# Who makes the low parts of the channel weights: VectorE or GpSimd, in a fused attention, gMLP and mixer kernel

## The chip, the cores and the metric

One NeuronCore of a Trainium2 chip. The metric is the device time of one launch in microseconds (us). Both versions take the same inputs and compute the same outputs.

## The reference, cut to what matters

Three stages follow each other over 4 batches of 576 tokens. The change touches the last half of the last one, and the end of the one before it.

```python
# 1: windowed attention, 8 heads of 64 -> x [4, 576, 512]
# 2: gMLP (moe_*), gives x again as [4, 576, 512]
# 3: mixer (moe2_*)
xt = x.transpose(0, 2, 1)
h = np.maximum(xt @ w_tok1, 0.0) @ w_tok2           # token layers: 576 -> 256 -> 576
u = x + h.transpose(0, 2, 1)
h2 = np.maximum(u @ w_ch1, 0.0) @ w_ch2             # channel layers: 512 -> 1536 -> 512
return (u + h2).astype(np.float32)                  # the residual is u
```

## The kernel before, in words

**Products in three passes.** A float32 operand is kept as two float32r parts: the high part is a rounded copy that ScalarE makes, the low part is the raw value minus the high one. A product is three matmuls (high by high, high by low, low by high), `product` in the code.

**Stages.** Attention, gMLP and the token layers run batch by batch, by orders written out by hand for each engine (`PROLOGUE_`, `FIRST_`, `LOOP_`, `EPILOGUE_`). In them `b00` to `b31` are the eight pieces of the second token layer, and `te` is VectorE's addition of x to a piece. VectorE then transposes the sum in 32 by 32 blocks (`ut0` to `ut3`), and SyncE stores it twice: `st` as it is, for the channel layers' input, and `sr` as rows, for the final residual (four issues for each of four pieces).

**The channel stage.** It runs over the 2304 tokens in NS = 3 spans of 768, and in each span over NI = 6 blocks of hidden channels, so NW = 18 rounds n = 0 to 17; s and i are the span and the block of round n. A round has seven first products P0 to P6 (`first_product`, six matmuls of 128x384 each). They are a Strassen-like scheme: seven products of sums of quarters in place of eight. Then there are twelve second products (`second_product`, three matmuls of 128x512 each), which add into six PSUM banks over the six rounds of a span. TensorE runs the first products of round n and puts the second products of round n - 1 behind them, 2, 2, 2, 1, 2, 2 and 1 of them after P0 to P6 (`AFTER_SLOT`).

**What each round needs.** SyncE loads the channel weights: `load_weights(n + 1)` (three issues, first product, waits for P6 of round n - 1) and `load_second(n)` (one issue, second product). VectorE's `weight_sums` makes four sums of quarters (L1162 to L1167), ScalarE's `weight_high` (L879) the high parts of all seven, 1792 elements per partition, and `second_high` (L883) those of the second weights, 1024 elements. GpSimd makes the low parts: `second_low` (L729, 1024) and `weight_low` (L725, 1792). For the next span's tokens, `data_sum` (VectorE), `data_high` (ScalarE) and `data_low` (GpSimd, L718, 768 elements) do the same, seven times per span.

**The products' results.** PSUM bank 6 is copied out by ScalarE (`copy_part` 0, 1, 2, L887, after P0, P2, P4), and VectorE's `add_part` 0, 1, 2 (L1173) adds bank 7 to such a copy. P3 waits for `add_part` 0, P6 for `add_part` 1, P1 of the next round for `add_part` 2. P2, P4 and P5 each wait for a `copy_part`. ReLU and the split into high and low parts are `hidden_high` j (ScalarE, L895, L899) and `hidden_low` j (VectorE, L1178), j = 0 to 3. P0 of the next round waits for `hidden_low` 2, since it writes the same bank.

**The end of a span.** At i = 0 the six output tiles of the span before are ready one after the other. `add_rest` r to r + 5 (VectorE, L1187) adds the residual rows to a tile, SyncE's `store` writes it out and `load_rest` fetches the next residual rows into one of three buffers; those of r + 3, r + 4 and r + 5 are loaded only after `add_rest` of r, r + 1 and r + 2. The second products of the new span start each bank anew, so the first of them waits for `add_rest` r + 3, the second for r + 4, the third for r + 5.

**The order.** Each engine runs its instructions in program order, so an instruction that waits holds all behind it on its engine. SyncE issues all DMAs, in one order too.

## Time and profile before

| | us |
|---|---|
| median of 3 runs | 674.92 |
| lowest, highest | 674.79, 676.52 |
| the profiled execution | 676.68 |
| its span, first to last instruction | 674.7 |

| engine | busy, share of the span |
|---|---|
| TensorE | 643.8 us, 95% |
| VectorE | 403.8 us, 60% |
| ScalarE | 297.8 us, 44% |
| GpSimd | 272.9 us, 40% |

### The profile page before, as it was taken

What the parts mean: (1) busy time and instruction counts of PE and PEld (TensorE: products, weight loads), DVE (VectorE), ACT (ScalarE), POOL (GpSimd) and SP (SyncE); (2) the same over time, 40 slices, a digit from 0 to 9 for tenths busy, and PEclk for the clock granted to TensorE, in tenths of its full rate; (3) what the DMA queues carried; (4) which work ended last, traced back from release to release, by engine and by line L of the source; (5) the groups of instructions that cost most, each with busy time, mean ns of one, the idle gap of its engine ahead of it and who ended that gap; (6) DMA issues with size and microseconds to landing.
All of it is one profiled execution on the core that took longest, in us unless ns stands there. A gap on an engine that the chain in (4) does not pass through costs nothing.

```text
span 674.7 us, 11567 instructions
## 1 busy us (share of the span) xinstructions
PE 643.8 (95%) x3917; PEld 590.7 (88%) x3917; DVE 403.8 (60%) x1026; ACT 297.8 (44%) x733; POOL 272.9 (40%) x279
## 2 busy tenths in 40 slices
PE   5999999999999999999999789999899999899995
PEld 5898999999999999999999678998788989789893
DVE  4987977578766786656645366445665435344422
ACT  4965357334563354633363235543244543333320
POOL 3551536412153121541058034686153776154310
PEclk9999999999999999999999889999999999999998
DMA  9868144585436863347211731324522323522314
GB/s 203 204 113 184 32 131 125 125 175 122 120 95 133 182 129 91 102 130 153 86 32 39 218 103 63 110 63 164 194 63 62 111 63 93 173 63 62 110 32 140
DMA packets 190873, 77.49 MB, mean 115 GB/s; under 512 B 127328, under 2 KB 177056, under 8 KB 190816
## 3 DMA queue, kind: packets, MB, share of 16 engines
q1 hardware_dynamic: 190816, 76.76, 44.1%
q8 instruction: 32, 0.52, 0.3%
q14 instruction: 25, 0.20, 0.1%
HBM read 55.49 MB, written 21.23 MB: 114 GB/s over the span
## 4 chain that ended last, share of the span: by engine, by line
PE 84%; DMA 4%; DVE 4%; issue 3%; SPq 2%; ACT 1%; POOL 0%; DVEq 0%; POOLq 0%
PE ps L1277 59%; PE ps L1378 13%; PE ps L1347 5%; PE ps L1317 5%; DMA front<-in_moe_w_ch_dram 1%; DMA early<-u_rows 1%; PE ps L1441 1%; SPq L579 1%; DMA xT<-u_scratch 1%; DVE arena L1178 1%; DVE att L1001 1%; PE ps L1327 1%; DVE front L1187 0%; ACT xT L887 0%; DVE att L1154 0%
## 5 line engine op out<-in xcount | busy, mean ns | idle before, releaser
L1277 PE MATMUL ps<-arena 128*128 128x288 f32 (+3 forms) x2100 | 399.2, 344 | 4.2 <-ACT xT L887 2.6
L1277 PEld LDWEIGHTS ps<-arena 128*128 128x128 f32 (+1 forms) x2100 | 336.0, 187 | 40.1 <-issue 5.2
L1277 PE MATMUL ps<-att_r,arena 128*128 128x384 f32 x504 | 102.3, 339 | 9.7 <-ACT xT L887 5.8
L1277 PEld LDWEIGHTS ps<-att_r,arena 128*128 128x128 f32 x504 | 90.5, 189 | 18.7 <-issue 11.9
L729 POOL TENSOR_TENSOR arena<-front,arena 128x1024 fp32r<-128x1024 f32 x18 | 44.3, 2458 | 146.7 <-ACT arena L883 146.7
L687 POOL TENSOR_SCALAR att<-att,rinv 128x128 f32<-128x128 f32 x144 | 53.2, 389 | 97.9 <-DVE rinv L1012 97.7
L1378 PE MATMUL ps<-arena 128*128 128x288 f32 (+1 forms) x560 | 89.6, 316 | 0.0
L1378 PEld LDWEIGHTS ps<-arena 128*128 128x128 f32 x560 | 80.5, 188 | 4.1
L725 POOL TENSOR_TENSOR arena<-front,arena 128x1792 fp32r<-128x1792 f32 x18 | 74.7, 4149 | 0.0
L1173 DVE TENSOR_TENSOR vr<-ps,xT 128x384 f32<-128x384 f32 x36 | 20.0, 556 | 87.2 <-ACT xT L887 54.0
L789 ACT ACTIVATE att<-att,nmax 128x128 f32<-128x128 f32 x144 | 56.0, 391 | 25.0 <-DVE nmax L1001 24.4
L899 ACT ACTIVATE arena<-vr 128x384 fp32r<-128x384 f32 x36 | 18.9, 526 | 67.2 <-PE ps L1277 46.1
L1178 DVE SCALAR_TENSOR_TENSOR arena<-vr,arena 128x384 fp32r<-128x384 f32 x36 | 40.3, 1121 | 9.7 <-ACT arena L899 9.7
L887 ACT ACTIVATE xT<-ps 128x384 f32<-128x384 f32 x54 | 26.2, 485 | 42.0 <-PE ps L1277 41.9
L1001 DVE CUSTOM_DVE_ANT_0 att<-ps,mask 128x128 f32<-128x128 f32 x144 | 33.1, 285 | 10.7 <-PE ps L1317 10.1
L718 POOL TENSOR_TENSOR att_r<-att,att_r 128x768 fp32r<-128x768 f32 x14 | 26.8, 1933 | 30.9 <-DVE att L1157 30.9
L1317 PE MATMUL ps<-att 128*128 128x128 f32 x288 | 37.5, 280 | 1.2 <-DVE att L975 1.2
L1347 PE MATMUL ps<-att 128*128 128x128 f32 x288 | 36.9, 276 | 0.7 <-DVE att L975 0.4
L1317 PEld LDWEIGHTS ps<-att 128*128 128x128 f32 x288 | 35.5, 197 | 1.6 <-DVE att L975 1.4
L693 POOL TENSOR_TENSOR rstd<-veps,mhalf 128x1 f32<-128x1 f32 (+1 forms) x20 | 12.7, 637 | 58.3 <-DVE veps L1077 58.3
L1347 PEld LDWEIGHTS ps<-att 128*128 128x128 f32 x288 | 34.8, 192 | 1.4 <-DVE att L975 0.6
L799 ACT ACTIVATE xT<-ps 64x256 f32<-64x256 f32 x72 | 27.1, 376 | 14.6 <-PE ps L1347 13.6
(98 smaller groups left out, 665.9 us busy)
## 6 DMA issues: line engine op xcount, KB each, us to landing
front<-in_moe_w_ch_dram SPq DMA_DIRECT2D x18, 512.0 KB, 4.8
prob_blocks<-att SPq DMA_DIRECT2D x27, 256.0 KB, 2.5
att<-prob_blocks SPq DMA_DIRECT2D x108, 64.0 KB, 2.0
u_scratch<-uy SPq DMA_DIRECT2D x16, 288.0 KB, 2.8
front<-in_moe_w_ch_dram SPq DMA_DIRECT2D x18, 256.0 KB, 2.9
front<-in_moe_w_ch_dram SPq DMA_DIRECT2D x36, 128.0 KB, 3.3
early<-u_rows SPq DMA_DIRECT2D x18, 256.0 KB, 4.5
att<-in_v_dram SPq DMA_DIRECT2D x16, 256.0 KB, 3.8
```

Source lines behind the costliest of these rows:

```text
L687: ins = pool.tensor_scalar(x, x, rinv[:, g % 3, p:p + 1], 1.0, ALU.mult, ALU.mult)
L718: pool.tensor_tensor(x_at[s % 2][:, c, 1], x_raw[s % 2][:, c, 1], x_at[s % 2][:, c, 0].bitcast(F32), ALU.subtract) \
L725: pool.tensor_tensor(a_lo_at[n % 2], a_raw[n % 2], a_hi_at[n % 2].bitcast(F32), ALU.subtract).then_inc(a_lo, 1)
L729: pool.tensor_tensor(w2_lo_at[n % 2], w2_raw[n % 2], w2_hi_at[n % 2].bitcast(F32), ALU.subtract).then_inc(w2_lo, 1)
L789: ins = act.activation(x, x, ACT.Exp, bias=nmax[:, g % 3, p:p + 1], scale=-1.0, accum_out=psums[:, g % 3, p:p + 1])
L799: ins = act.activation(xT3[c, :, blk * WINDOW:(blk + 1) * WINDOW], tp[c, bank, :].rearrange("p (w h n) -> p w h n", w=PAIRS, h=2)[:, :, h, ...
L1001: ins = dve.tensor_tensor_reduce(out=prob[:, g % 3, P * p:P * (p + 1)], in0=ps[:, 4 + g % 2, P * p:P * (p + 1)], in1=mask[:, 0:P] if blk e ...
L1178: dve.scalar_tensor_tensor(out=h_at[:, j, 1], in0=src, scalar=0.0, in1=h_at[:, j, 0].bitcast(F32), op0=ALU.max, op1=ALU.subtract).then_inc ...
L1277: ins = pe.matmul(dst, w[a], x[c], start=first and n == 0, stop=last and n == 2, skip_group_check=True)
L1317: ins = pe.matmul(ps[:, 4 + g % 2, P * p:P * (p + 1)], qd[:, g // 2 % 2, g % 2, p].rearrange("p h n -> p (h n)"), kT[:, p, at:at + P], sta ...
L1347: ins = pe.matmul(tp[:, bank, P * p:P * (p + 1)], window[:, P * p:P * (p + 1)], keys[:, p], start=True, stop=True)
L1378: ins = pe.matmul(dst, d, w, start=t == 0 and n == 0, stop=t == NT - 1 and n == len(pairs) - 1, skip_group_check=True)
```

## The change

1. `weight_low` and `second_low` of rounds from 1 on (for the weights of rounds from 2 on) go from GpSimd to VectorE, with semaphores of their own (`a_low`, `w2_low`). GpSimd keeps `data_low`, and in the opening the low parts of the first weights.
2. Within a round the order on VectorE and ScalarE is written anew: `second_high` stands behind `copy_part` 2 rather than ahead of `copy_part` 1; `hidden_low` 0 stands ahead of `weight_sums`; `data_sum` comes one block later (i = 2, 3) and `data_high` is spread as 2, 2, 2 and 1; `add_rest` comes later in the round at i = 0.
3. At the end of the last batch (`EPILOGUE_`), TensorE puts P2 to P6 of round 0 between the pieces b of the second token layer rather than behind them, and VectorE and ScalarE follow; the transposes `ut` come last on VectorE.
4. SyncE issues the second weights of round 1 (`cw41`) ahead of the stores `st3`, and the first weights of round 2 (`ca42`) behind them but ahead of the row stores `sr3`. Before, both came after all stores, in the loop.

The diff:

```diff
--- before.py
+++ after.py
@@ -67,7 +67,7 @@
         "V7 V8 b21 v2 + b31 v3 + v4 + u00 + u10 + u20 + u30 + u01 + u11 + u21 + u31 +").split()
     EPILOGUE_PE = (
         "g00 + g10 + g20 + g30 + g01 + g11 + g21 + g31 + y00 + y10 + y20 + y30 + y01 + t0 t1 y11 + y21 + y31 + a0 "
-        "t2 t3 a1 t4 a2 a3 a4 P0 P1 b00 b10 b20 b30 b01 b11 b21 b31 P2 P3 P4 P5 P6").split()
+        "t2 t3 a1 t4 a2 a3 a4 P0 P1 b00 P2 b10 P3 b20 P4 b30 b01 P5 b11 P6 b21 b31").split()
     PROLOGUE_ACT = (
         "qe0 qe1 e0 e1 qe2 e2 e3 o0 e4 o1 xh0 qe3 o2 e5 e6 wh0 o3 xh1 ze4 wh1 wh2 o4 e7 o5 e8 xh2 vr0 vr1 wh3 o6 "
         "o7 xh3 uu00 vh0 vr2 uu10 o8 uu20 xh4 vh1 vh2 uu30 wh4 vr3 vr4 wh5 vh3 uu01 vh4 uu11 uu21 uu31").split()
@@ -81,7 +81,7 @@
         "uu20 uu30 uu01 uu11 vh4 uu21 uu31").split()
     EPILOGUE_ACT = (
         "gh00 gh10 gh20 gh30 ae0 gh01 xe0 gh11 yy00 xe1 yy10 yy20 gh21 gh31 xe2 yy30 xe3 yy01 th0 th1 xe4 yy11 "
-        "yy21 xe5 yy31 we0 th2 th3 th4 ae1 xe6 ah0 ah1 pc0 pc1 pc2 he0 he1 he2 he3").split()
+        "yy21 xe5 yy31 we0 th2 th3 th4 ae1 xe6 ah0 ah1 pc0 he0 pc1 pc2 he1 he2 he3").split()
     PROLOGUE_DVE = (
         "ke0 m0 vo1 m1 r0 ke1 ke2 r1 m2 c0 hu0 m3 r2 c1 m4 vo2 r3 c2 m5 ke3 hv0 hv1 hv2 r4 c3 m6 xl0 lv0 hu1 hv3 "
         "c4 r5 r6 lv2 m7 wl0 c5 m8 xl1 vo3 r7 wl1 wl2 c6 xl2 hu2 r8 hu3 c7 vs0 vs1 wl3 vo4 vn0 xl3 c8 vl0 vn1 vs2 "
@@ -99,8 +99,8 @@
         "te30 te01 vn0 vs1 te11 vl0 te21 te31 vn1 ut0 vs2 ut1 vl1 vn2 vs3 vl2 vn3 ut2 ut3 vs4 kt0 vl3 vn4 kt1 vl4").split()
     EPILOGUE_DVE = (
         "sa00 sm00 gl00 sa10 sm10 gl10 sa20 sm20 sa30 gl20 as0 sm30 xs0 gl30 sa01 sa11 sm01 gl01 sm11 sa21 gl11 "
-        "sa31 xs1 sm21 sm31 xs2 gl21 gl31 as1 xs3 tl0 tl1 tl2 tl3 tl4 al0 al1 cs0 te00 te10 te20 te30 te01 te11 "
-        "te21 te31 ut0 ut1 ut2 cs1 ut3 cs2 dh0 dh1 dh2 dh3").split()
+        "sa31 xs1 sm21 sm31 xs2 gl21 gl31 as1 xs3 tl0 tl1 tl2 tl3 tl4 al0 al1 te00 cs0 te10 dh0 te20 te30 te01 "
+        "cs1 te11 dh1 dh2 cs2 te21 te31 dh3 ut0 ut1 ut2 ut3").split()
     PROLOGUE_POOL = (
         "n0 n1 lu0 n2 n3 lv1 n4 lv3 n5 n6 lu1 n7 lu2 n8 lu3 rs0 rs1 rs2 rs3 rs4").split()
     FIRST_POOL = (
@@ -117,7 +117,7 @@
         "pr22 pw23 pr23 lv22 pw24 pr24 lv23 pw25 pw26 pr25 pr26 lv24 pw27 pw28 pr27 pr28 lk30 st10 st11 st12 st13 "
         "lq30 sr10 lv30 sr11 sr12 sr13 lv31 pw30 pw31 pr30 pr31 pw32 pr32 pw33 pr33 lv32 pw34 pr34 lv33 pw35 pw36 "
         "pr35 pr36 lv34 pw37 pw38 pr37 pr38 st20 cx40 st21 sr20 st22 cx41 sr21 st23 sr22 sr23 cx42 ca40 ca41 cx43 "
-        "cw40 st30 sr30 sr31 sr32 sr33 st31 st32 st33").split()
+        "cw40 cw41 st30 st31 st32 st33 ca42 sr30 sr31 sr32 sr33").split()
     SEGMENTS = {"PE": [PROLOGUE_PE, FIRST_PE, LOOP_PE, LOOP_PE, EPILOGUE_PE], "ACT": [PROLOGUE_ACT, FIRST_ACT, LOOP_ACT, LOOP_ACT, EPILOGUE_ACT],
                 "DVE": [PROLOGUE_DVE, FIRST_DVE, LOOP_DVE, LOOP_DVE, EPILOGUE_DVE],
                 "POOL": [PROLOGUE_POOL, FIRST_POOL, LOOP_POOL, LOOP_POOL, EPILOGUE_POOL]}
@@ -347,6 +347,8 @@
         w2_in = [sem(f"w2_in{i}") for i in range(2)]
         w2_hi = sem("w2_hi")
         w2_lo = sem("w2_lo")
+        a_low = sem("a_low")
+        w2_low = sem("w2_low")
         xc_in = [sem(f"xc_in{i}") for i in range(2)]
         xc_sum = sem("xc_sum")
         xc_hi = sem("xc_hi")
@@ -607,6 +609,8 @@
                     load_data(0, x)
                 elif kind == "ca":
                     sp.wait_ge(*unit_full(("u", B - 1, 31)))
+                    if x == 2:
+                        sp.wait_ge(first_done, 7)
                     load_weights(x)
                 elif kind == "cw":
                     sp.wait_ge(*unit_full(("g", B - 1, 31)))
@@ -631,12 +635,11 @@
                 sp.dma_start(rows_out[at:at + P, :], osb[r % 4]).then_inc(o_stored[r % 4], 16)
 
             for n in range(1, NW + 1):
-                if n + 1 < NW:
+                if 2 < n + 1 < NW:
                     sp.wait_ge(first_done, 7 * n)
                     load_weights(n + 1)
-                if n < NW:
-                    if n >= 2:
-                        sp.wait_ge(second_done, 12 * (n - 1))
+                if 2 <= n < NW:
+                    sp.wait_ge(second_done, 12 * (n - 1))
                     load_second(n)
                 if n == 1:
                     sp.wait_ge(*unit_full(("acc_a", B - 1, KT - 1)))
@@ -746,14 +749,9 @@
                 else:
                     piece_low(kind[1:], b, x)
 
-            for n in range(1, NW):
-                s, i = divmod(n, NI)
-                second_low(n)
-                if n + 1 < NW:
-                    weight_low(n + 1)
-                if s + 1 < NS:
-                    for k in ((), (), (), (0, 1), (2, 3, 4), (5, 6))[i]:
-                        data_low(s + 1, k)
+            for s in range(1, NS):
+                for k in range(7):
+                    data_low(s, k)
 
         @block.scalar
         def _(act):
@@ -939,17 +937,19 @@
             for n in range(1, NW):
                 s, i = divmod(n, NI)
                 copy_part(n, 0)
+                if s + 1 < NS:
+                    for k in ((), (), (), (0, 1), (2, 3), (4, 5))[i]:
+                        data_high(s + 1, k)
+                if i == 0:
+                    data_high(s, 6)
                 hidden_high(n, 0)
-                second_high(n)
                 copy_part(n, 1)
                 if n + 1 < NW:
                     weight_high(n + 1)
                 copy_part(n, 2)
+                second_high(n)
                 hidden_high(n, 1)
                 hidden_high(n, 2)
-                if s + 1 < NS:
-                    for k in ((), (), (0, 1), (2, 3, 4), (5, 6), ())[i]:
-                        data_high(s + 1, k)
                 hidden_high(n, 3)
 
         @block.vector
@@ -1165,6 +1165,14 @@
                 dve.tensor_tensor(raw[:, 4], raw[:, 3], raw[:, 0], ALU.subtract).then_inc(a_sum, 1)
                 dve.wait_ge(a_sum, 4 * n + 3)
                 dve.tensor_tensor(raw[:, 6], raw[:, 1], raw[:, 4], ALU.subtract).then_inc(a_sum, 1)
+
+            def weight_low(n):
+                dve.wait_ge(a_hi, n + 1)
+                dve.tensor_tensor(a_lo_at[n % 2], a_raw[n % 2], a_hi_at[n % 2].bitcast(F32), ALU.subtract).then_inc(a_low, 1)
+
+            def second_low(n):
+                dve.wait_ge(w2_hi, n + 1)
+                dve.tensor_tensor(w2_lo_at[n % 2], w2_raw[n % 2], w2_hi_at[n % 2].bitcast(F32), ALU.subtract).then_inc(w2_low, 1)
 
             def add_part(n, x):
                 dve.wait_ge(part_copied, 3 * n + (1, 3, 2)[x])
@@ -1240,35 +1248,35 @@
                 elif kind[0] == "l":
                     piece_low(kind[1:], b, x)
 
-            for n in range(1, NW + 1):
+            for n in range(1, NW):
                 s, i = divmod(n, NI)
                 r = 6 * (s - 1)
-                if n < NW:
-                    add_part(n, 0)
-                    if n + 1 < NW:
-                        weight_sums(n + 1)
-                    hidden_low(n, 0)
-                if s + 1 < NS and i in (1, 2):
-                    data_sum(s + 1, 2 * i - 2)
-                    data_sum(s + 1, 2 * i - 1)
+                add_part(n, 0)
+                hidden_low(n, 0)
+                if n + 1 < NW:
+                    weight_sums(n + 1)
+                if s + 1 < NS and i in (2, 3):
+                    data_sum(s + 1, 2 * i - 4)
+                    data_sum(s + 1, 2 * i - 3)
+                if n + 1 < NW:
+                    weight_low(n + 1)
+                add_part(n, 1)
                 if i == 0:
                     add_rest(r)
-                if n < NW:
-                    add_part(n, 1)
+                    add_rest(r + 1)
+                hidden_low(n, 1)
+                hidden_low(n, 2)
                 if i == 0:
-                    add_rest(r + 1)
                     add_rest(r + 2)
-                if n < NW:
-                    hidden_low(n, 1)
-                    hidden_low(n, 2)
+                    add_rest(r + 3)
+                second_low(n)
+                add_part(n, 2)
+                hidden_low(n, 3)
                 if i == 0:
-                    add_rest(r + 3)
                     add_rest(r + 4)
-                if n < NW:
-                    add_part(n, 2)
-                    hidden_low(n, 3)
-                if i == 0:
                     add_rest(r + 5)
+            for r in range(6 * (NS - 1), 6 * NS):
+                add_rest(r)
 
         @block.tensor
         def _(pe):
@@ -1470,7 +1478,10 @@
             def first_product(n, k):
                 bank = ps[:, 6 + SLOT_BANK[k], 0:CK]
                 if k == 0:
-                    pe.wait_ge(a_lo, n + 1)
+                    if n < 2:
+                        pe.wait_ge(a_lo, n + 1)
+                    else:
+                        pe.wait_ge(a_low, n - 1)
                     apart(pe)
                     if n == 0:
                         for u in TP[-2:]:
@@ -1502,7 +1513,10 @@
                     pe.wait_ge(h_lo, 4 * n + j + 1)
                     apart(pe)
                 if u == 0:
-                    pe.wait_ge(w2_lo, n + 1)
+                    if n == 0:
+                        pe.wait_ge(w2_lo, 1)
+                    else:
+                        pe.wait_ge(w2_low, n)
                     apart(pe)
                 if n == 0 and u < 6:
                     if bank in (4, 5):
```

## Rows read from the trace of the kernel before

**Rows 1.** the page's busy line: busy us, share of the span, instructions

```profile
PE 643.8 (95%) x3917; PEld 590.7 (88%) x3917; DVE 403.8 (60%) x1026; ACT 297.8 (44%) x733; POOL 272.9 (40%) x279
```

**Rows 2.** TensorE's waits in the channel stage: us in total, times, longest

```profile
PE ps L1277 <- ACT xT L887: 8.4, 4, 2.7
PE ps L1277 <- DVE arena L1178: 3.2, 3, 2.1
```

**Rows 3.** timeline of TensorE, opening: start, us, instruction [idle before <- releaser]

```profile
357.77 2.27 PE L1277 MATMUL ps<-att_r,arena 128*128 128x384 f32 x12
359.88 6.52 PE L1277 MATMUL ps<-arena 128*128 128x288 f32 x48
366.24 3.29 PE L1277 MATMUL ps<-att_r,arena 128*128 128x384 f32 x18
370.20 2.32 PE L1277 MATMUL ps<-att_r,arena 128*128 128x384 f32 x12 [0.67 <-ACT xT L887]
374.67 1.56 PE L1277 MATMUL ps<-att_r,arena 128*128 128x384 f32 x6 [2.14 <-DVE arena L1178]
...
388.26 1.53 PE L1277 MATMUL ps<-att_r,arena 128*128 128x384 f32 x6 [2.75 <-ACT xT L887]
...
396.49 1.30 PE L1277 MATMUL ps<-att_r,arena 128*128 128x384 f32 x6 [1.55 <-DVE vr L1173]
...
398.32 1.22 PE L1277 MATMUL ps<-att_r,arena 128*128 128x384 f32 x6
```

**Rows 4.** two-us windows: busy by engine, PEclk (granted clock), DMA share, GB/s

```profile
376.00:378.00 2.00, 2.00 (x6) 1.61 (x6) 0.00 (x0) 0.49 (x1) 0.00 (x0) 0.50 0.82 205
...
586.00:588.00 2.00, 0.00 (x0) 0.00 (x0) 0.89 (x2) 1.40 (x3) 0.26 (x1) 1.00 0.02 6
```

**Rows 5.** timeline of TensorE: round 12, and the last second products

```profile
560.59 1.22 PE L1277 MATMUL ps<-att_r,arena 128*128 128x384 f32 x6
...
574.54 1.20 PE L1277 MATMUL ps<-att_r,arena 128*128 128x384 f32 x6
...
576.28 1.22 PE L1277 MATMUL ps<-att_r,arena 128*128 128x384 f32 x6
...
657.29 9.04 PE L1277 MATMUL ps<-arena 128*128 128x512 f32 x39
```

**Rows 6.** timelines of SyncE and VectorE around the loads for round 2

```profile
367.61 6.46 SPq L579 DMA_DIRECT2D u_rows<-early  x12
...
380.41 0.38 SPq L591 DMA_DIRECT2D front<-in_moe_w_ch_dram  x1
...
385.32 0.42 DVE L1162 TENSOR_TENSOR front<-front 128x256 f32<-128x256 f32 x1 [4.77 <-DMA front<-in_moe_w_ch_dram]
```

**Rows 7.** single lines: durations in ns, min/median/max

```profile
L1162 DVE TENSOR_TENSOR front<-front x18: 415/424/427, 330.0 to 630.9; 128x256 f32<-128x256 f32 x18
...
L1149 DVE TENSOR_TENSOR att<-xT,att x2: 949/950/951, 331.8 to 487.9; 128x768 f32<-128x768 f32 x2
L1149 DVE TENSOR_TENSOR early<-xT,early x1: 4244/4244/4244, 390.8 to 390.8; 128x768 f32<-128x768 f32 x1
...
L725 POOL TENSOR_TENSOR arena<-front,arena x18: 4041/4070/4793, 349.1 to 636.1; 128x1792 fp32r<-128x1792 f32 x18
...
L729 POOL TENSOR_TENSOR arena<-front,arena x18: 2389/2408/3097, 366.2 to 648.3; 128x1024 fp32r<-128x1024 f32 x18
```

**Rows 8.** timelines of ScalarE, VectorE and TensorE in rounds 12 and 13

```profile
567.32 1.69 ACT L879 ACTIVATE arena<-front 128x1792 fp32r<-128x1792 f32 x1
...
571.55 0.56 DVE L1173 TENSOR_TENSOR vr<-ps,xT 128x384 f32<-128x384 f32 x1 [1.01 <-ACT xT L887]
...
576.95 0.69 DVE L1187 TENSOR_TENSOR front<-ps,early 128x512 f32<-128x512 f32 x1 [1.89 <-DMA early<-u_rows]
...
588.19 1.28 PE L1277 MATMUL ps<-att_r,arena 128*128 128x384 f32 x6 [2.42 <-ACT xT L887]
```

**Rows 9.** timeline of SyncE, round 12, one load of residual rows

```profile
573.12 0.43 SPq L626 DMA_DIRECT2D early<-u_rows  x1
```

## The prediction

> **What bounds the kernel now.** I read the busy line first: TensorE is busy 95% of the span, VectorE 60%, GpSimd 40% [rows 1]. Moving work between the last two can pay only where it ends a wait of TensorE. So next its waits: in the channel stage (from 366 us) they are nearly all behind a ScalarE copy, L887 (8.4 us), and VectorE's L1178 and L1173 [rows 2]; the timeline says where. A round without waits takes 576.28 - 560.59 = 15.69 us [rows 5]; a first product takes 2.11 / 2 = 1.05 (two from 357.77 to 359.88) [rows 3], a second product 9.04 / 13 = 0.695 [rows 5]. With P0 at 0 that puts P1 at 2.4, P3 at 7.3, P4 at 9.1, P5 at 11.5, P6 at 13.95, P0 of the next round at 15.7 and its first second product at 16.7. Excess over this pace:
>
> - Opening, 357.77 to 398.32 (P0 of round 2): 40.55 us. The work is seven first products (7.35), the b pieces (366.24 - 359.88 = 6.36) and one round (15.69): 29.4. Excess 11.1. Its waits are 0.67, 2.14, 2.75 and 1.55, 7.1 in all [rows 3]; most of the rest is TensorE at 1.2 GHz behind two of them (granted 0.50 at 376) [rows 4].
> - Rounds 2 to 11: 560.59 - 398.32 - 156.9 = 5.4 us excess [rows 3, 5], at the first change of span (rounds 6 to 8).
> - From P0 of round 13 to the last matmul: 657.29 + 9.04 - 576.28 = 90.05 us, against five rounds and twelve second products, 78.45 + 8.34: 3.25 excess [rows 5], 2.42 of it the wait of P4 in round 13 [rows 8].
>
> The other rounds have nothing to give.
>
> **The opening.** P2 to P6 of round 0 now have pieces of b between them (0.8 us each), which cover the copy, addition and split that each waits for. I follow the queues: P5 comes at about 367.1, P6 at 368.95, b31 ends at 371.5. `hidden_low` 2 of round 0 needs P5's end (368.2), then ScalarE and VectorE at about 0.5 us an instruction behind `te11` and `hidden_low` 1: ready about 370.2. P0 of round 1 then starts at 371.5 without a wait, not at 374.67. One possible hitch, `hidden_low` 0 against GpSimd's running subtraction, costs VectorE up to 1.8 us near 363 and nothing on TensorE.
>
> In round 1 the wait of 2.75 at P4 is the copy queued behind `second_high`, whose load SyncE issued only after the row stores (6.46 us for twelve of sixteen) [rows 6]. `cw41` is now issued before all stores, and `second_high` is behind the copy: gone. The wait of 1.55 at P6 is `add_part` 1 behind `data_sum`, which waited for its load and then took 4.24 us beside GpSimd instead of 0.95 [rows 7]. `data_sum` now comes in rounds 2 and 3: gone. What is late next: the first weights of round 2. `ca42` follows `st33`, which needs `te31` (372.2), so it is issued at 372.7 and lands, at the 4.9 us seen before (380.41 to 385.32) [rows 6], at 377.6. From there: sums 4 x 0.42 [rows 7], `weight_high` 1.7 [rows 8], and `copy_part` 2 behind it must be out by P5 at 383.0. That allows sums from 379.1: 1.5 us to spare. The transposes (3 us on VectorE) end at 375.5, before `add_part` 0 is wanted (P3 at 378.8). The sixteen row stores occupy SyncE until 383.3 and delay the token load; the weights of round 3 land behind it at about 393, and 394.8 is early enough. So P0 of round 2 is at 371.5 + 15.7 = 387.2: 11.1 us gained, bounded by 6 (one or two waits of the old sizes come back, with the low clock) and 11.1.
>
> **The steady rounds.** No row has VectorE subtracting 1792 elements. From 256 to 768 it goes from 424 to 950 ns, 1.03 ns per element [rows 7]: by that line 2.0 us and, for 1024, 1.2 us. From below, the 0.95 us of 768 is a floor; from above, GpSimd's 4.07 and 2.41 [rows 7]. I take the line, since both its points are the same operation on the same engine. `add_part` 0 starts when P1 ends (3.7), `hidden_high` 0 and `hidden_low` 0 follow to 5.6, the four sums take to 7.2 and `weight_high` to 8.9 (1.7) [rows 8]; `weight_low` 8.9 to 10.9; `add_part` 1 then starts at 10.95, and before it started at 571.55 - 560.59 = 10.96 [rows 8], because it waits for P4's copy. So it is just covered; P6 wants it at 13.95. `second_high` ahead of `hidden_high` 1 moves that to 11.8, `hidden_low` 2 ends at 13.9 (P0 wants it at 15.7), `second_low` at 15.1 (wanted at 16.7). Cost nothing, with 1.6 to 2.4 us of cover. GpSimd's relief (4.07 + 2.41 us a round) [rows 7] gives nothing either: nobody waited for it in a steady round. In the rounds at i = 3, two `data_low` and two `data_sum` are added: `hidden_low` 0 stands still for about 1.6 us, `add_part` 1 ends at 13.1, `hidden_low` 2 at 14.85, `second_low` at 16.1. Cover falls to 0.6 us, still nothing.
>
> The Trainium skill (SBUF — State Buffer, "SBUF: two separate sides") says that VectorE's two-SBUF-input instructions and GpSimd's lock one another out for whole instructions, and this speaks against moving such work to VectorE. The trace agrees: 0.95 us became 4.24 [rows 7]. By that rule every new subtraction may stand still for one `data_low`; since only seven of those per span are left, the sum stays. The skill's VectorE: DVE Perf Modes ("The TRN2 errata") has a formula that gives 2.02 and 1.22 us for the two subtractions.
>
> **The changes of span (rounds 6 to 8, 12 to 14).** Here I expect a trade, not a gain. Old waits that go: P4 of rounds 7 and 13, behind `second_high` (2.42 at 588.19) [rows 8], and what followed. New: at i = 0 VectorE now runs `add_rest` r only after `add_part` 1, at 11.5 (ends 12.15), and its successor's load goes out behind it at 12.6. `add_rest` r + 3 needs that load, which takes at least 3 and up to 4.2 us (one issued at 573.12 was waited for until 576.95) [rows 8, 9]: 15.7 to 16.8. Behind it on VectorE are `second_low`, `add_part` 2, `hidden_low` 3, `add_rest` r + 4. So `second_low` ends at 17.6 to 18.4, and the first second product waits 1 to 1.7 us. `hidden_low` 3 must have `add_part` 2 and ScalarE first, so `add_rest` r + 4 ends at 20.1 to 20.8, and the second of the second products, planned for 17.4, waits for it. Loss 2.7 to 3.5 us per change. Then the weights of round 8 or 14 are issued behind the last store at about 21.2, and the waits they can cause are just covered by the later plan (0.4 us to spare, so up to 0.5 more). Together 6 to 8 us for both, against 5.4 + 3.25 = 8.65 now: gain 1.3, bounds +2.6 and -3.
>
> Whether so split a wait lowers the clock is open: it fell after waits of 2.14 and 2.75 us in the opening, but not at 586 to 588 with no matmul at all in those 2 us [rows 4]. One drop costs about 1.5 us, from the opening's 11.1 - 7.1 = 4.0 over two. I count half of two drops less what the restart already costs: 1 us off. The skill (TensorE: Matmul & The Clock Gate, "HAM oscillation") ties the drop to idle gaps long enough; with both new waits below the old 2.75 it would predict none, and the sum would be 1 us lower.
>
> **Sum.** Opening 11.1, changes of span 1.3 - 1.0 = 0.3, steady and tail 0: 11.4. The profiled execution took 676.68 with a span of 674.7, so 665.3 with 663.3; it lay 1.76 above the median of 674.92. Against the median: 663.5.
>
> **The rivals.**
> - A: the changes of span get worse, 3.5 + 0.5 + 1.5 us each with a clock drop, 11 against 8.65, and more if the residual rows land late. For it: VectorE is held with `second_low` queued behind. Gain 8 to 9: 666.5.
> - B: a load takes the place of the wait in the opening: `ca42`'s weights land after 379.1, or round 3's after 394.8, because row stores in small pieces share the DMA engines. Two to four us of wait with the low clock: 667.5. Against it: 1.5 us to spare at both.
> - C: the residual rows are there in time and the changes of span cost nothing: up to 8 us more gain, 656 to 660. Against: the load is issued behind `add_rest` r, whose place I know.
> - D, the other side: VectorE becomes the bound of every round. At GpSimd's prices `weight_low` ends at 13, `hidden_low` 2 at 15.3, `second_low` at 17.7, 1.0 us late in each of 16 rounds: 16 lost against 11.4 gained, 679.5. It decides from 0.7 us a round, which needs 3.8 us for `weight_low` (2.1 ns per element, twice the line). Against: the line of rows 7. Lockouts in the rounds with GpSimd work would feed it, but those are six.
>
> **How the numbers follow.** Forecast 0.66 (own range 661 to 666), A 0.12, B 0.09, C 0.06, D 0.05, other 0.02. The range 659.5 to 668.5 takes in A, B and the near part of C and the bounds of the open terms. A measurement here tells about 0.3% (2 us) from no change: faster 0.91 (all but D and half of the rest), same 0.03, slower 0.06.
>
> **What the profile would show.** Right: TensorE without a gap from 357.8 to about 387, granted clock 1.00 there; L725's and L729's successors on VectorE at 2.0 and 1.2 us; two waits behind VectorE right at the first second products of rounds 6 and 12 (run in rounds 7 and 13), none at P4. Wrong: P5 or P6 waiting in ordinary rounds (D), P5 in round 1 or 2 behind L879 (B), or a lower clock at 475 or 575 (A).

## The result, and the profile after

| | before | changed |
|---|---|---|
| median of 4 runs, us | 675.4 | 664.88 |
| lowest, highest | 674.79, 676.52 | 663.9, 668.81 |
| profiled execution, its span | 676.68, 674.7 | 668.81, 666.0 |

The ratio is 0.9848 (95% interval 0.981 to 0.9887). Five more runs of the same kernel beside other runs of before gave 664.91 and 0.9827 (0.9804 to 0.9851). Forecast was 663.5, in 659.5 to 668.5. The profiled execution is the slowest of the nine; where it matters I use the second profile too, with a span of 662.5.

The page's line that answers to [rows 1], and the group of the moved subtraction (out<-in, count | busy us, mean ns | idle before and its releaser):

```profile
PE 642.8 (97%) x3917; PEld 591.7 (89%) x3917; DVE 426.6 (64%) x1059; ACT 298.0 (45%) x733; POOL 167.6 (25%) x246
...
L1171 DVE TENSOR_TENSOR arena<-front,arena 128x1792 fp32r<-128x1792 f32 x16 | 32.4, 2025 | 21.3 <-ACT arena L877 21.2
```

GpSimd's busy time falls by 105 us. VectorE takes 2.03 us for what took GpSimd 4.07, and its two new groups are busy for 55 us; its total still rises by 23 only, since most of the lockouts between the two engines are gone and its other work takes 32 us less. TensorE's work is the same to 1 us; what changed is when it waits. The timeline of TensorE after, against [rows 3] and [rows 5]:

```profile
359.34 2.27 PE L1285 MATMUL ps<-att_r,arena 128*128 128x384 f32 x12
...
373.11 1.22 PE L1285 MATMUL ps<-att_r,arena 128*128 128x384 f32 x6
...
388.80 1.22 PE L1285 MATMUL ps<-att_r,arena 128*128 128x384 f32 x6
...
401.35 1.28 PE L1285 MATMUL ps<-att_r,arena 128*128 128x384 f32 x6 [0.88 <-ACT xT L885]
471.02 0.92 PE L1285 MATMUL ps<-arena 128*128 128x512 f32 x3 [1.45 <-DVE arena L1175]
473.15 79.67 PE L1285 MATMUL ps<-arena 128*128 128x512 f32 x381 [1.20 <-DVE front L1195]
570.76 0.93 PE L1285 MATMUL ps<-arena 128*128 128x512 f32 x3 [1.19 <-DVE arena L1175]
572.89 0.98 PE L1285 MATMUL ps<-arena 128*128 128x512 f32 x3 [1.20 <-DVE front L1195]
649.00 9.04 PE L1285 MATMUL ps<-arena 128*128 128x512 f32 x39
```

From P0 of round 0 (359.34) to P0 of round 2 (388.80) it is 29.46 us, where it was 40.55. The 0.88 us in round 2 is P5 behind `weight_high`, whose weights came late. Every other ordinary round runs without a wait. Then two waits stand at each change of span, at the first and the second of the second products: `second_low` (L1175) and `add_rest` r + 4 (L1195). VectorE's timeline there (round 6) shows why:

```profile
463.62 0.56 DVE L1181 TENSOR_TENSOR vr<-ps,xT 128x384 f32<-128x384 f32 x1
464.09 1.28 DVE L1195 TENSOR_TENSOR front<-ps,early 128x512 f32<-128x512 f32 x2
...
466.41 0.68 DVE L1195 TENSOR_TENSOR front<-ps,early 128x512 f32<-128x512 f32 x1
469.05 0.69 DVE L1195 TENSOR_TENSOR att<-ps,early 128x512 f32<-128x512 f32 x1 [1.97 <-DMA early<-u_rows]
469.66 1.22 DVE L1175 TENSOR_TENSOR arena<-front,arena 128x1024 fp32r<-128x1024 f32 x1
470.79 0.55 DVE L1181 TENSOR_TENSOR xT<-ps,xT 128x384 f32<-128x384 f32 x1
471.94 0.56 DVE L1186 SCALAR_TENSOR_TENSOR arena<-xT,arena 128x384 fp32r<-128x384 f32 x1 [0.59 <-ACT arena L897]
472.41 1.39 DVE L1195 TENSOR_TENSOR front<-ps,early 128x512 f32<-128x512 f32 x2
```

`add_rest` r + 3 waits 1.97 us for residual rows, and `second_low`, `add_part` 2, `hidden_low` 3 and `add_rest` r + 4 stand behind it.

**One scale for all kernels.** Without a wait, TensorE needs 13.8 us for the opening's products, 17 rounds of 15.69 and the last 8.34, 288.8 us from P0 of round 0 to the last matmul. The excess over that, and the tail from the last matmul to the end of the span:

| kernel | excess us | tail us |
|---|---|---|
| before | 19.8 | 8.4 |
| changed, first and second profile | 9.9, 8.8 | 8.0, 6.9 |
| e1_opening | 20.9 | 7.1 |
| e2_loop | 13.2 | 7.3 |
| e3_lows_on_gpsimd | 14.9 | 7.7 |
| e6_opening_late_sums | 12.5 | 7.2 |
| e7_double_low | 19.2 | 7.9 |
| e9_before_six_rest | 16.7 | 4.3 |
| e10_late_sums_six_rest | 8.4 | 4.3 |
| e4_six_rest | 2.9 | 3.4 |
| e5_rest_order, e8_best | 0.0, 0.0 | 3.5, 3.5 |

(For the changed kernel: 649.00 + 9.04 - 359.34 - 288.8 = 9.9.) From the starts of P0 in each round, the excess of the changed kernel lies in three places. In the first profile it is 1.1 us in round 2, 5.9 at the first change of span and 2.9 at the second; in the second profile it is 0, 2.9 and 6.0. Before, it was 11.1 in the opening and 5.4 and 3.3 at the changes of span. P0 of round 0 itself starts between 357.0 and 359.6 us in the thirteen profiles, without order; that is not the change's.

### The profile page after: what moved, and what is told of

It is laid out like the page before. It is cut to its first block, busy times and chain, and to the rows that moved or that the text cites. A ratio compares the mean times of both kernels' runs of the same rounds, so it can differ in the third digit from the quotient of the medians.

```text
span 666.0 us, 11552 instructions
## 1 busy us (share of the span) xinstructions
PE 642.8 (97%) x3917; PEld 591.7 (89%) x3917; DVE 426.6 (64%) x1059; ACT 298.0 (45%) x733; POOL 167.6 (25%) x246
## 4 chain that ended last, share of the span: by engine, by line
PE 87%; DMA 5%; DVE 3%; SPq 2%; issue 1%; ACT 1%; POOL 1%; DVEq 0%; POOLq 0%; ACTq 0%
PE ps L1285 63%; PE ps L1386 13%; PE ps L1355 4%; PE ps L1325 4%; DMA early<-u_rows 2%; DMA early<-in_moe_w_spatial_dram 2%; PE ps L1449 1%; SPq L581 1%; DMA front<-in_moe_w_ch_dram 1%; DVE front L1195 1%; PE ps L1304 0%; PE ps L1374 0%; DVE arena L1171 0%; DMA u_rows<-gate 0%; DVE att L1001 0%
## 5 line engine op out<-in xcount | busy, mean ns | idle before, releaser
L1171 DVE TENSOR_TENSOR arena<-front,arena 128x1792 fp32r<-128x1792 f32 x16 | 32.4, 2025 | 21.3 <-ACT arena L877 21.2
L1186 DVE SCALAR_TENSOR_TENSOR arena<-vr,arena 128x384 fp32r<-128x384 f32 x36 | 25.8, 718 | 23.6 <-ACT arena L897 23.6
L877 ACT ACTIVATE arena<-front 128x1792 fp32r<-128x1792 f32 x18 | 30.7, 1703 | 16.6 <-DVE front L1167 16.6
L897 ACT ACTIVATE arena<-xT 128x384 fp32r<-128x384 f32 x18 | 9.5, 525 | 53.0 <-PE ps L1285 29.8
```

The source lines that it names most:

```text
L877: act.activation(a_hi_at[n % 2], a_raw[n % 2], ACT.Copy).then_inc(a_hi, 1)
L897: act.activation(h_at[:, j, 0], total[i], ACT.Relu).then_inc(h_hi, 1)
L1171: dve.tensor_tensor(a_lo_at[n % 2], a_raw[n % 2], a_hi_at[n % 2].bitcast(F32), ALU.subtract).then_inc(a_low, 1)
```

## The experiments

Each has four to twelve runs, beside runs of before with medians of 676.8, 676.5 and 676.9 us in the three batches. The edits are cut to what matters, and words stand for the longer ones.

### e1: the opening alone

```diff
 the orders EPILOGUE_PE, _ACT, _DVE and ALL_SP, and SyncE's loop: as changed
 GpSimd's, ScalarE's and VectorE's loops: as before
```

> Only the opening of the change: the interleaved orders of the last batch and the early weight loads; the loop is that of before (GpSimd makes the low parts). My theory: the opening and the loop's new order need each other. P0 of round 1 comes 3.2 us earlier and at full clock, P4 of round 1 no longer waits, but data_sum still stands ahead of add_part 1 in round 1, and the token load behind the row stores lands no earlier than about 392 us, so P6 of round 1 waits some 7 to 9 us in place of 1.55. Time 672 to 675. Rival (the parts are independent, each wait goes by itself): 675.4 - 9.5 = about 666.

676.63 us, ratio 1.0004 (0.9982 to 1.0026). TensorE's timeline in round 1:

```profile
395.41 2.26 PE L1278 MATMUL ps<-att_r,arena 128*128 128x384 f32 x6 [9.47 <-DVE vr L1174]
```

VectorE in front of it:

```profile
392.97 0.96 DVE L1150 TENSOR_TENSOR early<-xT,early 128x768 f32<-128x768 f32 x1 [11.89 <-DMA xT<-u_scratch]
```

The whole gain of the opening is given back in one wait. P6 of round 1 waits 9.47 us for `add_part` 1, queued behind a `data_sum` that waits for tokens loaded behind the row stores: they are issued at 385.56 us, 3.1 later than before. The clock is at 1.2 GHz for 10 us around it. The theory held in its mechanism; the wait was half a microsecond longer than the 7 to 9 that I gave it, and the time 1.6 us above my range of 672 to 675.

### e2: the loop alone

```diff
 the three loops, a_low and w2_low: as changed
 the EPILOGUE_ orders, ALL_SP and SyncE's loop: as before
```

> Only the loop of the change: the new orders within a round and the low parts on VectorE; the opening and SyncE's order are those of before. My theory: the waits of 0.67 and 2.14 us in the opening and the low clock behind them stay; round 1's 2.75 us at P4 turns into about 1.5 us at P5, behind the weight copy whose weights still land at 385 us; the 1.55 us at P6 goes. About 4.5 us gained in the opening, changes of span as in the changed kernel: 669 to 672. Rival (the move of work between engines brings nothing by itself, all of the gain is in the opening's order): 675.

671.65 us, ratio 0.992 (0.9898 to 0.9942). As expected the opening's own waits stay, and round 1 has one of 0.97 where 2.75 and 1.55 were:

```profile
369.99 2.32 PE L1284 MATMUL ps<-att_r,arena 128*128 128x384 f32 x12 [0.67 <-ACT xT L884]
374.45 1.97 PE L1284 MATMUL ps<-att_r,arena 128*128 128x384 f32 x6 [2.14 <-DVE arena L1185]
388.72 1.28 PE L1284 MATMUL ps<-att_r,arena 128*128 128x384 f32 x6 [0.97 <-ACT xT L884]
```

The two halves are worth 0 and 5 us alone and 11 together.

### e6: the opening with late data sums

```diff
 e1, and in VectorE's loop:
-                if s + 1 < NS and i in (1, 2):
-                    data_sum(s + 1, 2 * i - 2)
-                    data_sum(s + 1, 2 * i - 1)
+                if s + 1 < NS and i in (2, 3):
+                    data_sum(s + 1, 2 * i - 4)
+                    data_sum(s + 1, 2 * i - 3)
```

> The kernel of e1 (opening alone, the loop of before, GpSimd makes all low parts), with one more edit: data_sum one block later, in rounds 2 and 3 of a span. My theory: the 9.5 us wait at P6 of round 1 in e1 is data_sum's wait for the token load and nothing else, so this one edit gives the whole opening back; the old changes of span stay (8 us): 11 us under before less about 1 for the late weights of round 3, 664 to 667, the time of the full change, with no work moved to VectorE. Rival (the low parts must go to VectorE for the gain): 670 or more.

669.14 us, ratio 0.9894 (0.9875 to 0.9912): 2 us slower than the top of what I expected. The 9.47 us is gone, so `data_sum` was its cause, and 7 us of gain come with no work moved. What I had too small is the wait in round 2:

```profile
388.35 1.30 PE L1278 MATMUL ps<-att_r,arena 128*128 128x384 f32 x6 [0.24 <-DVE arena L1179]
399.53 2.16 PE L1278 MATMUL ps<-att_r,arena 128*128 128x384 f32 x6 [1.87 <-ACT xT L888]
...
482.87 6.85 PE L1278 MATMUL ps<-arena 128*128 128x384 f32 x33 [2.41 <-ACT xT L888]
...
580.43 2.16 PE L1278 MATMUL ps<-att_r,arena 128*128 128x384 f32 x6 [2.51 <-ACT xT L888]
```

With `second_high` ahead of `copy_part` 1, the late load is that of the second weights (landed at 397.93), and it costs P4, 2.4 us earlier in the round than P5: 1.87 us with 3.4 us of low clock behind it, in place of the changed kernel's 0.88. Round 2 lost 3.8 us in all, where I had taken 1.

### e3: the low parts back on GpSimd

```diff
             add_part(n, 0) ... weight_sums(n + 1) ... data_sum
-            weight_low(n + 1)
             ...
-            second_low(n)
 GpSimd, every round:
+            data_low of the round; weight_low(n + 1); second_low(n)
```

> The changed kernel with weight_low and second_low of the rounds back on GpSimd, all orders otherwise as changed. My theory: which engine makes the low parts is worth little, since steady rounds have cover either way: the changes of span get about 1 us each cheaper (second_low is no longer behind add_rest), rounds 2 and 3 of each span lose up to 0.6 us each to lockouts between the two engines. Time within 2 us of the changed kernel, 663 to 667. Rival (the engine move is what pays, since GpSimd locks VectorE out for 4 us in every round): over 670.

671.16 us, ratio 0.9911 (0.9891 to 0.993), against 0.9848 and 0.9827 for the change: I was wrong and the rival right on the time, by 4 to 6 us. TensorE and GpSimd, around round 3:

```profile
420.92 1.28 PE L1289 MATMUL ps<-att_r,arena 128*128 128x384 f32 x6 [1.50 <-POOL arena L728]
423.42 1.62 PE L1289 MATMUL ps<-arena 128*128 128x512 f32 x6 [1.21 <-POOL arena L732]
```

```profile
412.67 3.65 POOL L721 TENSOR_TENSOR arena<-early,arena 128x768 fp32r<-128x768 f32 x2 [8.26 <-DVE early L1164]
416.28 4.35 POOL L728 TENSOR_TENSOR arena<-front,arena 128x1792 fp32r<-128x1792 f32 x1
420.59 2.68 POOL L732 TENSOR_TENSOR arena<-front,arena 128x1024 fp32r<-128x1024 f32 x1
```

But not by the rival's mechanism. GpSimd's 4.07 and 2.41 us are longer by 0.3 each here, which I put down to lockouts; what costs is its own queue. `data_low` waits for the fourth `data_sum` of this very round, at 412.6, and the two of them, `weight_low` and `second_low` then follow one another: 10.7 us, past the 419.4 us at which P0 wants its weights. I had let `data_low` start as soon as its high part was there. The waits in rounds with data, 0.51, 1.50 and 1.21 in one span and 0.50, 1.50 and 1.19 in the next, sum to 6.4 us. One part of the theory held: the waits at the changes of span are 1.21 and 1.54 us, in place of 2.65 and 2.39.

This run has one order of GpSimd's queue, `data_low` first. With the `data_low` behind the two others, `weight_low` could run from 412.4, when `weight_high` ends, to 416.5 and `second_low` to 419.2, before 419.4. That is an estimate from this trace; no run tests it.

### e7: one more subtraction on VectorE in rounds 4 to 16

```diff
             def weight_low(n):
                 dve.wait_ge(a_hi, n + 1)
+                if n >= 5:
+                    dve.tensor_tensor(<unused memory>, a_raw[n % 2], a_hi_at[n % 2].bitcast(F32), ALU.subtract)
```

> The changed kernel with one subtraction of weight_low's size more on VectorE ahead of weight_low, into unused memory, in rounds 4 to 16 (13 times 2.0 us). Asks how much cover VectorE has left. My theory: in ordinary rounds add_part 1 moves from 10.96 to 12.9 in the round and P6 still starts on time, second_low ends at 16.4, wanted at 16.7: no wait there; about 1.4 us is lost in the two i = 3 rounds less (only round 9 in the second span) and up to 2 us at each change of span: 3 to 6 us slower than the changed kernel, 668 to 671. Rival D of the prediction (VectorE is as good as the bound): 13 x 2 us, over 685.

676.02 us, ratio 0.9988 (0.9973 to 1.0003), some 10 us over the change: twice what I expected (3 to 6), and far from the 26 of rival D, 13 times 2 us. All of TensorE's waits from round 4 on:

```profile
433.10 1.28 PE L1288 MATMUL ps<-att_r,arena 128*128 128x384 f32 x6 [0.34 <-DVE vr L1184]
449.80 1.30 PE L1288 MATMUL ps<-att_r,arena 128*128 128x384 f32 x6 [0.80 <-DVE vr L1184]
470.99 1.46 PE L1288 MATMUL ps<-arena 128*128 128x512 f32 x3 [2.45 <-DVE arena L1178]
473.11 46.06 PE L1288 MATMUL ps<-arena 128*128 128x512 f32 x216 [0.66 <-DVE front L1198]
520.13 16.36 PE L1288 MATMUL ps<-arena 128*128 128x384 f32 x78 [0.96 <-DVE vr L1184]
537.31 15.94 PE L1288 MATMUL ps<-arena 128*128 128x384 f32 x78 [0.82 <-DVE vr L1184]
554.01 1.98 PE L1288 MATMUL ps<-arena 128*128 128x384 f32 x9 [0.75 <-DVE vr L1184]
575.47 0.93 PE L1288 MATMUL ps<-arena 128*128 128x512 f32 x3 [2.77 <-DVE arena L1178]
577.59 1.65 PE L1288 MATMUL ps<-arena 128*128 128x512 f32 x3 [1.19 <-DVE front L1198]
```

No wait stands in rounds 6, 8, 12 and 14 to 16, nor in rounds 7 and 13 behind the two at the change of span: there the 2.0 us are covered, as I said. The new waits stand in every round with `data_low` (i = 3, 4 and 5), not at i = 3 alone, because a VectorE subtraction now meets a `data_low` there. By the starts of P0 these rounds lose 5.3 us, and the changes of span lose 5.1 more than in the first profile of the change, 3 of that for a second stretch of low clock. The two engines' timelines in round 9:

```profile
514.17 7.04 POOL L721 TENSOR_TENSOR att_r<-att,att_r 128x768 fp32r<-128x768 f32 x2 [57.70 <-DVE att L1157]
```

```profile
513.91 2.02 DVE L1172 TENSOR_TENSOR uy<-front,arena 128x1792 f32<-128x1792 f32 x1
515.84 3.67 DVE L1174 TENSOR_TENSOR arena<-front,arena 128x1792 fp32r<-128x1792 f32 x1
```

GpSimd's pair takes 7.04 us instead of 3.65 and VectorE's second subtraction 3.67 instead of 2.02: they alternate, each standing still for the other (the two `data_low` take 3.47 and 3.62 us here, where one alone takes 1.84).

### e4, e5: rows in time, and a better order

```diff
-        rest = [early[...] for i in range(3)]
+        rest = [early[...] for i in range(3)] + [uy[...] for i in range(3)]
 load_rest: all six at n % 6 == 4, none between the stores
 e5 also:
                 second_low(n)
+                if i == 0: add_rest(r + 4)
                 add_part(n, 2)
+                if i == 0: add_rest(r + 5)
                 hidden_low(n, 3)
```

> The changed kernel with six buffers of residual rows in place of three, all loaded four rounds into a span, so that add_rest r + 3 waits for no load. Orders unchanged. My theory: at a change of span the first second product waits at most 0.1 us in place of 1.45 and 1.2, the second one still about 1.5 us for add_rest r + 4 behind hidden_low 3; one wait of 1.5 in place of two: 1 to 1.5 us gained per change, 661.5 to 663 by the median, and no drop of the clock. Rival (the two waits come from VectorE's load of work, not from the missing rows): no change, 664 to 665.

> The six-buffer kernel (e4_six_rest), and at i = 0 VectorE runs add_rest r + 4 ahead of add_part 2 and add_rest r + 5 ahead of hidden_low 3. My theory: the 0.83 us that the second of the second products still waits at each change of span goes, since only the queue on VectorE holds it: about 1.8 us less than e4, 653.3 (ratio to before about 0.966). Rival (add_part 2 is then late for P1 of the next round): a wait of the same size in another place, 655.

e4: 655.16 us, ratio 0.9685 (0.9668 to 0.9703), 9.7 us under the change where I expected 2 to 3. e5: 652.97 us, ratio 0.9662 (0.9643 to 0.9681), against the 653.3 expected. TensorE in e4:

```profile
400.95 1.28 PE L1283 MATMUL ps<-att_r,arena 128*128 128x384 f32 x6 [0.42 <-ACT xT L883]
470.70 76.95 PE L1283 MATMUL ps<-arena 128*128 128x512 f32 x381 [0.83 <-DVE front L1193]
565.92 0.97 PE L1283 MATMUL ps<-arena 128*128 128x512 f32 x3 [0.83 <-DVE front L1193]
```

The changes of span cost 0.83 us each, a little less than expected, and nothing in e5, whose timeline has no wait of TensorE from P0 of round 0 to the end (excess 0.0). What I had missed is the tail. VectorE there, in the changed kernel and in e4:

```profile
658.79 0.69 DVE L1195 TENSOR_TENSOR att<-ps,early 128x512 f32<-128x512 f32 x1 [2.06 <-DMA early<-u_rows]
661.54 0.69 DVE L1195 TENSOR_TENSOR front<-ps,early 128x512 f32<-128x512 f32 x1 [2.06 <-DMA early<-u_rows]
662.77 0.69 DVE L1195 TENSOR_TENSOR front<-ps,early 128x512 f32<-128x512 f32 x1 [0.54 <-DMA early<-u_rows]
```

```profile
649.76 0.69 DVE L1193 TENSOR_TENSOR att<-ps,uy 128x512 f32<-128x512 f32 x1
650.64 1.34 DVE L1193 TENSOR_TENSOR front<-ps,uy 128x512 f32<-128x512 f32 x2 [0.19 <-DMA out_dram<-front]
```

The last three rows' waits fall from 4.66 to 0.19 us. By the table e4 has 7.0 us less excess than the first profile of the change and 4.5 us less tail (5.9 and 3.5 against the second); 3 us of the excess is the low clock, which e4 and e5 do not show (granted 0.999 to 1.000).

### e8: the tokens of the second span loaded early

```diff
-        "... cw40 cw41 st30 st31 st32 st33 ca42 sr30 ..."
+        "... cw40 cw41 dx40 st30 st31 st32 st33 ca42 sr30 ..."     # dx: load_data(1, 0 to 3)
```

> e5_rest_order, and the tokens of the second span are loaded ahead of the stores of the last batch (they come from batches 1 and 2 and their place in SBUF is free once the first token layer of the last batch is done), so that the weights of round 3 no longer land behind them. My theory: the wait of P5 in round 2 (0.88 and 0.42 us in two profiles, behind the weight copy L877) goes: 0.5 to 1 us under e5, about 652.5, TensorE without a wait from 359 us on. Rival (the weights of round 3 are late for the sixteen row stores before them): no change against e5.

653.48 us (651.09 to 654.68), ratio 0.9657 (0.9634 to 0.9681): not to be told from e5, as the rival had it, where I expected 652.5. Both have no wait of TensorE in round 2; e5's weights of round 3 came in time without it, as in the second profile of the change, though VectorE waited 1.26 us for them there and not at all in e8. So the wait of 0.88 in the first one is a landing at the edge, and moving the tokens buys room, no time that can be measured. The row stores, which the rival named, are in e8 as well, and its weights are not late. The fastest single run is this kernel's.

### e9, e10: the six buffers on the old loop

> The kernel before with six buffers of residual rows, nothing else. My theory: the buffers are worth 4.5 us at the tail in any version (the last three add_rest no longer wait for loads), and little at the old changes of span, where the waits are the second weights' (P4 of rounds 7 and 13) - these shrink only since the last store, and with it the next weights, go out about 2 us earlier: 668.5 to 671. Rival (the buffers only help where VectorE queues second_low behind add_rest): 672 to 675.

> e6_opening_late_sums with six buffers of residual rows: the opening, late data sums and the buffers, all low parts on GpSimd in the old order of the loop. My theory: the tail's 4.5 us and part of the waits at the changes of span go from 669.1: 661 to 664, still 6 us or more over e4 and e5, because second_high ahead of copy_part 1 keeps its wait in round 2 and after each change of span. Rival (with rows in time GpSimd does as well): 656 or less.

e9 is before with the six buffers, e10 is e6 with them. 669.9 us, ratio 0.9898 (0.9875 to 0.9922), and 663.13 us, ratio 0.9785 (0.9761 to 0.9809): both times as I expected. The tail is 4.3 us in both. In e9 the way there was another than I wrote: the changes of span lose 4.8 us where they lost 8.7, a larger gain than the little that I had there, and the opening loses 0.9 more, with 5.21 us of wait at P4 of round 1 in place of 2.75 in this one profile. e10, with every low part on GpSimd, is a little under the full change (0.9827), and 8 and 10 us over e4 and e5 by the medians, 7 and 8 by the ratios. Its wait in round 2, at P4 behind `second_high`, is 2.50 us, and at each change of span 1.3.

### e11: the change again

> The changed kernel once more, five rounds, on the same chip as e9 and e10, to have its median beside theirs and to see whether the low clock after the change of span comes in every execution. My theory: 664 to 667; the granted clock in the profile differs from the first one's (0.990), since the fall behind the two waits of 1.45 and 1.20 us comes in some executions only. Rival: 668.8 with 0.990 as in the first profile, the fall belongs to the waits.

664.91 us (663.86 to 666.33). In the second profile the weights of round 3 landed in time for TensorE. VectorE's first sum of them, in the first profile and in the second:

```profile
397.53 0.42 DVE L1162 TENSOR_TENSOR front<-front 128x256 f32<-128x256 f32 x1 [3.14 <-DMA front<-in_moe_w_ch_dram]
```

```profile
394.75 0.43 DVE L1162 TENSOR_TENSOR front<-front 128x256 f32<-128x256 f32 x1 [1.68 <-DMA front<-in_moe_w_ch_dram]
```

The waits at the changes of span are the same to 0.4 us (1.09, 1.19, 1.47, 1.19). The low clock is not where it was. Windows of 2 us (columns as in [rows 4]) of the first profile of the change, and of the second:

```profile
474.00:476.00 2.00, 2.00 (x7) 1.81 (x7) 0.00 (x0) 0.00 (x0) 0.00 (x0) 0.50 0.84 286
...
574.00:576.00 2.00, 2.00 (x12) 1.78 (x11) 0.56 (x1) 0.26 (x1) 0.00 (x0) 1.00 0.89 283
```

```profile
474.00:476.00 2.00, 2.00 (x11) 1.78 (x10) 0.31 (x1) 0.49 (x1) 0.00 (x0) 1.00 0.85 164
...
570.00:572.00 2.00, 2.00 (x7) 1.81 (x7) 0.56 (x1) 0.00 (x0) 0.00 (x0) 0.50 0.92 246
```

Both of my alternatives were too plain: the clock fell once in each profile, behind the first change of span in the one and the second in the other, each time for 6.8 us. In both it was the change with the longer first wait (1.45 and 1.47 us, against 1.19 and 1.09). That does not settle it: in e3 the clock fell behind waits of 1.50 and 1.19 us at 523 and stayed at 2.4 GHz behind 1.50 and 1.21 at 423. What decides is open. By the starts of P0, a change of span costs 2.9 us without the low clock and 5.9 to 6.0 with it.

## Why the prediction was right, point by point

- **The opening, 11.1 us.** Right in size and in mechanism: 40.55 us became 29.46, P0 of round 1 came 13.77 us after P0 of round 0 (13.7 by the sum), the clock stayed at 2.4 GHz. e1 shows how narrow it was: with the token load where the change puts it, the old place of `data_sum` alone takes all of it back, and e6 that moving it is enough to have the gain. I had named both edits, not that one is the other's condition.
- **Late next.** The weights of round 2 landed in time. Those of round 3 I had landing at about 393, with 394.8 as early enough. Counted as in the prediction, from a P0 of round 0 at 357.77, they landed at 396.0 in the first profile and cost 1.1 us in round 2, 0.88 of it the wait of P5, rival B in small; in the second profile they landed at 394.5 and cost nothing. The limit was right; the landing was taken 1.5 to 3 us too early, and it was luck that so little came of it.
- **The steady rounds, 0.** Right. The line through 256 and 768 elements gave 2.0 and 1.2 us; measured 2.03 and 1.22 (2.04 for the two `second_low` in rounds 3 and 9, beside GpSimd's `data_low`). `add_part` 1 starts where it did: 463.62 in round 6, 10.96 us after P0. e7 measures the cover that was argued: 2.0 us more are free in rounds without `data_low`, and cost 0.3 to 1.0 us in rounds with it. Rival D was far off.
- **The lockouts.** The Trainium skill's rule that the loser stands still for the whole instruction (SBUF — State Buffer, "SBUF: two separate sides") is what e7 shows, 2.02 us becoming 3.67; in the change itself it cost TensorE nothing, as the sum had it.
- **What the engine move itself is worth.** The prediction gave it nothing, since nobody waited for GpSimd before. e3 shows 4 to 6 us: in the new order, with the queue that e3 gives GpSimd, its low parts are late. Beside that queue the move does not gain time, it keeps the new order from losing it. Whether another order on GpSimd would do as well is not shown: the estimate beside e3 says it could, and no run has the low parts on VectorE in the old order.
- **The changes of span.** The mechanism came out as written, two waits at the first and second of the second products, behind `second_low` and `add_rest` r + 4, and so did its times: in round 6 `add_rest` r + 3 starts 16.4 us after P0 (15.7 to 16.8 by the sum) and `second_low` ends at 18.2 (17.6 to 18.4). The waits are 2.65 and 2.39 us, and a change without the low clock loses 2.9, forecast 2.7 to 3.5. Two terms behind it were wrong and cancelled. The late weights of rounds 8 and 14 cost nothing, so both changes lose 5.8 us without the low clock, where 7.35 was taken. The clock fell for 6.8 us in each profile, twice as long as either stretch in the opening before (3.4), and cost 3.0 where the sum had 1. Together it is 8.8, where the sum had 8.35: that this term came out is half luck. Two steps of its working do not follow either: 4.0 us over two drops is 2.0 each and not 1.5, and the lower bound of 3 us lost does not come from 6 to 8 against 8.65.
- **The time.** The forecast takes 11.4 us off 674.92. The gain was 10.5 beside the four runs of before with 675.4, and 12.0 beside the eleven with 676.9. The 1.4 us by which 663.5 was low are within what separates such batches.
- **Tail, 0.** The change leaves it (8.4, then 8.0 and 6.9). Six buffers take 3.5 to 4.5 us off it, and I never looked: the last three additions waited 4.7 us for their rows.

## What to carry to other kernels

When a wait goes because a load is issued earlier, follow everything that the queue now issues later, and ask which instruction waits for it in its old place: here one edit was worth 0 us, the other 5, both 11. An engine that is busy for 64% of the span can still be the place of a wait, if an instruction that waits for a transfer stands ahead of the short links of the bounding engine's chain; more buffers, filled rounds ahead, took away most of two such waits, the low clock behind them and 3.5 to 4.5 us of tail, 9.7 us in all and nearly as much as the whole change. And look at the stretch behind the last matmul as closely as at the busy one.

## What the runs showed of the hardware that was not expected

- The clock fell after two waits of 1.45 and 1.20 us with three matmuls between them, to 1.2 GHz for 6.8 us, which cost 3.0, and did not fall after 1.19 and 1.20 us 100 us later; in the second profile it was the other way round, with 1.47 and 1.19 and with 1.09 and 1.19. The size of the waits does not decide it alone: e2 has the fall behind 1.03 and 1.19 us and none behind 1.25 and 1.20. In before it did not fall after single waits of 2.57 and 2.42 us at the changes of span, while in e1 it fell after 2.52 and 2.36 there. The Trainium skill (TensorE: Matmul & The Clock Gate, "HAM oscillation") ties the fall to long single gaps; here each gap was shorter than one that did no harm.
- A weight load issued at 389.06 us behind four token loads landed at 397.51, 8.5 us later, and 7.2 us in the second profile; the same load took 4.1 to 5.4 us in the other rounds of the stage.
- A subtraction of 1792 elements takes 2.03 us on VectorE and 4.07 on GpSimd; where both engines have several in a row (e7), they take turns and both lose: 2.02 became 3.67 us and 1.84 became 3.47 and 3.62.
